# Values before transposes in each attention step of TensorE

## What is computed

```python
scores = scale * np.matmul(q, k.transpose(0, 1, 3, 2))      # B=2, H=8, S=768, D=64
is_global = pos[None, :] < int(n_global)                    # 8
is_local = (rel >= 0) & (rel < int(n_local))                # 96
keep = is_global | is_local
scores = scores + bias[None, :, :, :]
scores = np.where(keep, scores, -1000000000.0)
scores = scores - np.max(scores, axis=-1, keepdims=True)
a = np.exp(scores)
a = a / (np.sum(a, axis=-1, keepdims=True) + 1e-09)
return np.matmul(a, v).astype(np.float32)
```

## Time and profile before

| | us |
|---|---|
| median of 3 runs | 512.72 (512.62 to 512.96) |
| profiled execution | 512.87 |
| its span, first to last instruction | 510.8 |
| attention on TensorE, last matmul of values followed by the next stage | 92.83 from the span's start |

### The profile page before, as it was taken

One profiled execution on the slowest core, in us unless ns is written; L12 is line 12 of the kernel. 1 busy time (PEld: TensorE's weight loads), 2 busy tenths in 40 slices (PEclk: granted clock), 3 DMA queues, 4 the chain that ended last, 5 costly groups with the idle time before them and its releaser, 6 DMA issues.

```text
span 510.8 us, 8127 instructions
## 1 busy us (share of the span) xinstructions
PE 504.8 (99%) x3049; PEld 471.6 (92%) x3049; DVE 258.1 (51%) x683; ACT 174.6 (34%) x371; POOL 142.6 (28%) x141
## 2 busy tenths in 40 slices
PE   8999999999999999999999999999999999999997
PEld 6999999889999999979999999988888899888897
DVE  7999998462111421264111425166775665754452
ACT  6999998421111111122111153313322321321130
POOL 3587775299800000005000050811300310000040
PEclk9999999999999999999999999999999999999999
DMA  7897774035300000003000011320000011000002
GB/s 234 315 311 238 247 223 165 5 125 184 112 33 1 0 2 0 1 1 124 1 0 1 0 63 62 129 80 0 1 1 2 0 63 62 1 1 0 1 31 94
DMA packets 10696, 37.20 MB, mean 73 GB/s; under 512 B 1312, under 2 KB 3360, under 8 KB 10656
## 3 DMA queue, kind: packets, MB, share of 16 engines
q1 hardware_dynamic: 10656, 36.67, 21.4%
HBM read 33.52 MB, written 3.15 MB: 72 GB/s over the span
## 4 chain that ended last, share of the span: by engine, by line
PE 97%; DVE 1%; DMA 1%; issue 1%; ACT 0%
PE bank L274 72%; PE bank L1383 7%; PE bank L1148 5%; PE bank L1178 4%; PE bank L1181 3%; PE bank L1162 2%; PE bank L1160 2%; PE bank L1239 1%; PE bank L1266 1%; DMA counts<-both_counts 1%; PE bank L1188 0%; DVE u_rows L1044 0%; ACT split L731 0%; DVE wsplit L809 0%; DVE wsplit L880 0%
## 5 line engine op out<-in xcount | busy, mean ns | idle before, releaser
L274 PE MATMUL bank<-hid,wsplit 128*128 128x384 f32 (+1 forms) x648 | 126.4, 344 | 0.1
L274 PEld LDWEIGHTS bank<-hid,wsplit 128*128 128x128 f32 x648 | 113.3, 188 | 3.9 <-issue 0.7
L274 PE MATMUL bank<-split,wsplit 128*128 128x384 f32 x576 | 108.1, 337 | 0.0
L274 PE MATMUL bank<-wsplit,zs 128*128 128x512 f32 (+1 forms) x576 | 104.1, 340 | 0.0
L274 PEld LDWEIGHTS bank<-wsplit,zs 128*128 128x128 f32 x576 | 89.1, 188 | 13.3
L274 PEld LDWEIGHTS bank<-split,wsplit 128*128 128x128 f32 x576 | 100.3, 188 | 0.0
L1054 DVE SCALAR_TENSOR_TENSOR hid<-bank,hid 128x384 fp32r<-128x384 f32 x48 | 26.7, 557 | 140.4 <-ACT hid L740 140.4
L585 POOL TENSOR_TENSOR wsplit<-wraw,wsplit 128x1536 fp32r<-128x1536 f32 (+1 forms) x18 | 58.6, 3262 | 75.3 <-ACT wsplit L701 74.4
L740 ACT ACTIVATE hid<-bank 128x384 fp32r<-128x384 f32 x48 | 23.6, 491 | 143.7 <-PE bank L274 143.7
L584 POOL CAST wsplit<-wraw 128x1536 fp32r<-128x1536 f32 (+1 forms) x12 | 15.9, 1323 | 136.3 <-PE bank L274 123.0
L517 POOL TENSOR_TENSOR wsplit<-qk_raw,wsplit 64x256 fp32r<-64x256 f32 x46 | 37.5, 815 | 26.2 <-DVE wsplit L817 25.3
(11 more groups left out here) (102 smaller groups left out, 583.7 us busy)
## 6 DMA issues: line engine op xcount, KB each, us to landing
wraw<-weights SPq DMA_DIRECT2D x16, 768.0 KB, 4.0
qk_raw<-qk SPq DMA_DIRECT2D x23, 528.0 KB, 4.8
vt<-v SPq DMA_DIRECT2D x10, 520.0 KB, 4.6
out<-act_raw SPq DMA_DIRECT2D x16, 192.0 KB, 1.9
wraw<-weights SPq DMA_DIRECT2D x4, 512.0 KB, 3.3
qk_raw<-qk SPq DMA_DIRECT2D x2, 264.0 KB, 3.5
vt<-v SPq DMA_DIRECT2D x2, 260.0 KB, 6.2
counts<-both_counts SPq DMA_DIRECT2D x1, 2.0 KB, 2.9
```

The costliest lines, as they stand in the source:

```text
L274: mm = pe.matmul(dst, lhs(a), rhs(c), start=first and i == 0, stop=last and i == 2, skip_group_check=True)
```

## The change

In TensorE's loop the two calls change places. In iteration m the values of step m - 3 now come right after the scores of step m (and the ones, where there are any), and the transposes of step m - 2 come last.

```diff
@@ -1197,10 +1197,10 @@
                     head_scores(m)
                 if m < len(FILL):
                     multiply_ones(FILL[m], [O_BANK[1]] * 2)
+                if 3 <= m < STEPS + 3:
+                    weigh_values(m - 3)
                 if 2 <= m < STEPS + 2:
                     transpose_probs(m - 2)
-                if 3 <= m < STEPS + 3:
-                    weigh_values(m - 3)
 
             general_tensor(pe, flag)
```

## The result

The changed kernel took **533.07 us** in the median of four executions (532.97 to 536.87), against 512.84 before (512.62 to 512.99, the three earlier executions and one more): slower by a factor of 1.041, 95% interval 1.039 to 1.043. The profiled execution took 533.13 us with a span of 531.0, which is 20.2 us more than the 510.8 of before.

What follows compares the result with a forecast made beforehand. TensorE was taken to bound the kernel; the reordered attention steps wait for ScalarE's copy. Terms 0.1, 9.1, 0.8, 10.5 and 0.05 sum to 20.5 us, giving 533.4 profiled, 533.2 us median, range 529 to 537.

Steps and rivals of the forecast that it cites:

- The hand-over: TensorE to ScalarE and back: last transpose to copy 0.31, copy 0.60, release of the values 0.05, sum 0.96 us.
- The step: Attention-stage cycle of values, next transposes, copy, next values: 2.24 us against 1.78, 0.46 us more per step.
- The cold start of the values: Values after a wait on TensorE take 0.95 us to the transposes; in flow 0.84, cycle 2.13, total about 529 us.
- The cover: TensorE work beside the copy's round trip: last transpose's slot 0.11 and scores 0.53, 0.64 us, leaving 0.32 bare per step.
- rival 2: Copy's round trip on TensorE covered, needing 0.96 to fall to 0.64: step stays 1.78, total 512.3 us; chance 0.03.
- The short steps: Values of steps 23 to 28, with short pieces at a batch's first row tile: 7.71 us against 6.94, +0.8.
- the start: Start of the attention stage: first full values come 0.1 us later than 19.50, +0.1.
- The end: End of the attention stage: next stage starts near 113.3 in place of 92.83, with 418 us unchanged from there.
- The load doesn't slip in front of the wait: Rival claimed TensorE's values load does go ahead of the wait: cycle 0.19 us shorter, total 525 us; chance 0.04.
- rival 3: VectorE joins the cycle, its keys delayed behind ScalarE's waiting copy: 20 steps at 2.5 us, total 538.5 us; chance 0.07.
- A lower clock for the whole stage: TensorE's clock falls throughout attention, doubling values and transposes: 55 us more, total 588 us; chance 0.03.
- The waits by row: Profile signs: values' loads wait about 43 times, nearly 0.45 us each, 19 in all; matmuls some 0.15, copies about 0.5.

## Why the prediction was right, point by point

- *The hand-over.* Worked out as 0.31 + 0.60 + 0.05 = 0.96 us, it is 49.77 to 50.73, 0.96. The rows it came from the earlier trace rows were places where the old kernel happened to wait as the new one does always.
- *The step.* 2.24 expected, 2.23 measured: from the first full values at 19.48 to those of step 23 at 61.89, 42.41 us in 19 steps, and the same 42.41 from 69.68 to 112.09. The cold start of the values was the right choice between the two ends.
- *The cover.* Given as 0.64 with 0.32 bare. It is 0.56: the scores start only 0.03 behind the last transpose, not 0.11, and 0.40 to 0.43 lies bare. This error had no effect, because the scores are not on the cycle, as the extra matmuls showed. In rival 2 the deciding point would have been 0.56.
- *The short steps.* 7.7 us expected for V(23) to V(28), 61.89 to 69.68 is 7.8; the start 0.1 later expected, 19.48 against 19.50 measured, nothing.
- *The end.* Expected at 113.3, measured at 113.01, and 418.0 us from there to the end of the span, as before. No large errors cancel in the sum: its five terms were 0.1, 9.1, 0.8, 10.5 and 0.05 and measured -0.02, 8.97, 0.85, 10.33 and 0.05, which gives 20.18. Not the last two but the last three steps have no scores; their period is 2.23 as well.
- *The rivals.* The load doesn't slip in front of the wait: the held row is the load's in all 44 waits. VectorE did wait for the keys, 10.8 us, as rival 3 describes, but it didn't join the cycle. The hand-over was not covered. A lower clock for the whole stage did not come; a short one did, in some executions. The reading of the earlier trace rows behind that rival is weaker than I wrote: the profile gives the granted clock as 1.00 between 4 and 6 us, where the slow pair of ones at 5.03 stands, so its 1.05 us is not shown to be the lower level by the granted clock.
- *The waits by row.* Each load of the values waits 19.7 / 44 = 0.45 us, as expected. The matmul row shows 11.3 / 41 = 0.28 each where I expected 0.15, and the copies wait 23.4 / 40 = 0.58 for the transposes where I expected 0.5. Neither is a term of the sum.
- *What was only half seen.* The sum gave the order no effect of its own on the step. It has a small good one, 0.05 us per step, that the wait hides.

## What to carry to other kernels

Where one engine's product goes through another engine and back, count the work between the two ends: start to start 0.31, the copy, and 0.05, against the instructions that stand between. Swapping two calls in a software pipeline changes that distance even if nothing is added; keep a whole step of distance, or shorten the copy. And to learn whether an engine is bound by its work or by a wait, add work there: here two matmuls a step cost 8.9 us in one order and nothing in the other.

## What the runs showed of the hardware that was unexpected

**The clock fell for some microseconds in some executions.** In the profiled execution of the changed kernel with six more matmuls the busy time by stretches of 2 us (length; PE, PEld, DVE, ACT, POOL; PEclk) reads:

```profile
116.00:118.00 2.00, 1.31 (x12) 1.08 (x12) 1.09 (x3) 1.47 (x5) 0.00 (x0) 1.00 0.00 0
118.00:120.00 2.00, 1.31 (x12) 1.08 (x12) 1.36 (x4) 1.12 (x3) 0.00 (x0) 1.00 0.00 0
120.00:122.00 2.00, 1.64 (x10) 1.24 (x9) 0.00 (x0) 0.32 (x1) 0.00 (x0) 0.59 0.00 0
122.00:124.00 2.00, 1.67 (x8) 1.68 (x9) 0.00 (x0) 0.27 (x1) 0.00 (x0) 0.50 0.04 8
124.00:126.00 2.00, 2.00 (x7) 1.61 (x7) 1.34 (x4) 0.63 (x1) 0.00 (x0) 0.50 0.00 0
126.00:128.00 2.00, 2.00 (x8) 1.57 (x7) 0.46 (x2) 0.63 (x1) 0.00 (x0) 0.70 0.01 4
```

From about 120 to 127 us the granted clock is 0.50, the 1.2 GHz of its two levels. The values there take about twice as long, 122.33 to 124.05, 1.7 us in place of the 0.92 of the earlier trace rows. Just before, TensorE's loads are busy for 1.08 of 2 us, in steps that consist of transposes, values and a bare hand-over, three in a row without scores. The changed kernel with two more matmuls shows the same in its profile, at 112 to 117 us. In the profiled execution of the changed kernel itself the same steps ran at 1.00 throughout. The steps inside the loop, with 33.81 of 42 us of loads, never showed it in a profile. I had given the lower clock a chance only for the whole stage, 55 us. What is seen is a mean clock of 0.990 to 0.997 in 3 of 9 executions of the changed kernel, which took 1.7 to 3.9 us more; where in these executions it fell, no profile shows. Nor is the end of the stage the only place. In the profile of the kernel with the longer distance it fell near the start:

```profile
12.00:14.00 2.00, 2.00 (x8) 1.70 (x8) 1.97 (x12) 1.63 (x6) 0.80 (x1) 0.50 0.54 116
```

That is the part of the program from which I had argued, by the earlier trace rows, that the clock stays up. It cost that execution nothing that can be told: 512.69 us, among others of the same kernel at a mean clock of 1.00 with 512.44 to 512.67. What decides in which execution the clock falls is open, and that the bare hand-overs at the end bring it down is likely but not proven.

**The order of the three pieces changes their price.** With every wait covered, scores, values, transposes take 1.19 + 0.84 + 0.36 = 2.39 us from start to start (with six more matmuls), and scores, transposes, values 1.20 + 0.44 + 0.81 = 2.45. The gain of 0.08 is at the seam behind the transposes: scores follow them after 0.36, values after 0.44; 0.03 of it is lost behind the values. The kernel with the longer distance shows the same without extra matmuls, 1.73 against 1.78. Why the one seam is shorter no run here shows.
